# Scores ahead of the hash steps, a split first tile, and an expert that waits block by block

## What is computed

```python
q_bits = (np.einsum('bhsd,dk->bhsk', q, proj) > 0)
k_bits = (np.einsum('bhsd,dk->bhsk', k, proj) > 0)
mask = q_bucket[:, :, :, None] == k_bucket[:, :, None, :]
scores = np.where(mask, scale * np.matmul(q, k.transpose(0, 1, 3, 2)), -1000000000.0)
attn = softmax(scores)          # minus the row's maximum, exp, divided by the row's sum
x = attn @ v                    # then 768 x 512
...
expert_idx = np.argmax(x @ w_gate, axis=1)       # 8 experts, at most 192 tokens each
h = np.maximum(np.einsum('ecd,edf->ecf', disp, w1), 0.0)
y = np.einsum('ecf,efd->ecd', h, w2)             # times the gate's weight
...
h = x @ w_in                                     # 512 -> 2048
out = (h * np.tanh(softplus(h))) @ w_out
```

## Time and profile before

| what | value |
|---|---|
| median of the runs | 420.18 us (419.67 to 420.54) |
| the profiled execution | 420.03 us, its span 418.2 us |
| PE busy | 402.1 us (96%) |
| DVE, ACT, POOL busy | 251.2, 200.5, 81.2 us |
| chain that ended last | PE 78%, DVE 13%, ACT 5%, issue 2%, DMA 1% |
| attention; experts; last network | 0 to 147 us; 158 to 280 us; 280 to 418 us |

### The profile page before, as it was taken

How to read it: one execution, slowest core, us unless ns; L and a number is a source line. 1 busy time by engine, 2 the same in 40 slices (tenths; PEclk the granted TensorE clock), 3 DMA queues, 4 the chain that set the end, 5 groups by cost and what they waited for, 6 DMA issues and landing times.

```text
span 418.2 us, 7265 instructions
## 1 busy us (share of the span) xinstructions
PE 402.1 (96%) x2675; PEld 369.2 (88%) x2677; DVE 251.2 (60%) x442; ACT 200.5 (48%) x388; POOL 81.2 (19%) x79
## 2 busy tenths in 40 slices
PE   8888999999999899999999999999999999999995
PEld 3567998998999788999999999999989899889984
DVE  4878889889999451201111011118899999777771
ACT  5867968968879311211011101106758564554441
POOL 1630320320600042084742600000000000000005
PEclk9999999999999989999999999999999999999999
DMA  8763931991600044999899899820000000000003
GB/s 297 251 126 87 267 75 39 303 201 40 239 2 0 2 162 148 407 388 320 302 380 344 327 371 350 330 92 2 0 2 0 2 2 2 0 0 2 0 2 150
DMA packets 15451, 62.85 MB, mean 150 GB/s; under 512 B 2112, under 2 KB 2752, under 8 KB 11328
## 3 DMA queue, kind: packets, MB, share of 16 engines
q1 hardware_dynamic: 14032, 58.51, 41.4%
q0 software_dynamic: 960, 3.15, 2.0%
q10 hardware_dynamic: 432, 0.83, 0.5%
HBM read 49.89 MB, written 3.15 MB: 127 GB/s over the span
## 4 chain that ended last, share of the span: by engine, by line
PE 78%; DVE 13%; ACT 5%; issue 2%; DMA 1%; POOLq 0%; POOL 0%; SPq 0%; DVEq 0%; ACTq 0%
PE ps L714 14%; PE ps L730 14%; PE ps L803 13%; PE ps L778 12%; PE ps L622 5%; PE ps L649 5%; PE ps L532 4%; DVE ptl L1160 3%; DVE nmax L1103 3%; PE ps L541 2%; PE ps L606 2%; PE ps L691 2%; PE ps L495 2%; ACT pth L926 1%; ACT prob L888 1%
## 5 line engine op out<-in xcount | busy, mean ns | idle before, releaser
L714 PE MATMUL ps<-xs,ring 128*128 x512 | 60.3, 278 | 1.9 <-issue 1.0
L714 PEld LDWEIGHTS ps<-xs,ring 128*128 128x128 f32 x512 | 58.6, 191 | 3.6 <-issue 3.5
L730 PE MATMUL ps<-hs,ring 128*128 128x128 f32 (+1 forms) x512 | 59.2, 276 | 0.0
L730 PEld LDWEIGHTS ps<-hs,ring 128*128 128x128 f32 x512 | 58.5, 192 | 0.0
L926 ACT ACTIVATE pth<-ps 128x384 fp32r<-128x384 f32 x96 | 42.2, 495 | 19.8 <-PE ps L649 19.3
L1160 DVE TENSOR_TENSOR ptl<-ps,pth 128x384 fp32r<-128x384 f32 x96 | 48.9, 551 | 3.6 <-ACT pth L926 3.5
L1103 DVE TENSOR_REDUCE nmax<-ps 128x1 f32<-128x768 f32 x48 | 45.7, 955 | 7.4 <-PE ps L532 5.9
L532 PE MATMUL ps<-ops 128*128 128x384 f32 x192 | 44.1, 352 | 1.4 <-ACT prob L888 1.4
L888 ACT ACTIVATE prob<-ps,nmax 128x768 f32<-128x768 f32 x48 | 43.5, 907 | 3.1 <-DVE nmax L1103 3.1
L649 PE MATMUL ps<-cfs,prob 128*128 128x128 f32 x288 | 41.3, 276 | 2.3 <-DVE ptl L1160 2.0
L778 PE MATMUL ps<-yh,wih 128*128 128x384 f32 x128 | 43.0, 336 | 0.3 <-ACT hc L1004 0.3
(11 more groups left out here) (160 smaller groups left out, 688.4 us busy)
## 6 DMA issues: line engine op xcount, KB each, us to landing
ring<-in_w SPq DMA_DIRECT2D x32, 1024.0 KB, 6.8
winraw<-in_w_in SPq DMA_DIRECT2D x8, 512.0 KB, 5.9
woutraw<-in_w_out SPq DMA_DIRECT2D x8, 512.0 KB, 6.7
ops<-kh SPq DMA_DIRECT2D x12, 192.0 KB, 3.5
ops<-qh SPq DMA_DIRECT2D x6, 384.0 KB, 5.7
xg<-rows SPq DMA_DIRECT2D x1, 1539.0 KB, 8.7
raw<-in_vt SPq DMA_DIRECT2D x4, 384.0 KB, 5.2
raw<-in_qt SPq DMA_DIRECT2D x3, 384.0 KB, 6.7
```

The lines of the kernel that those rows point to most:

```text
L714: last = mm(ps[:, fc // 2, (fc % 2) * WIDE:(fc % 2) * WIDE + W], wa[:, 2 * fc // KF, kd, P * (fc % (KF // 2)):P * (fc % (KF // 2)) + P], x ...
L730: last = mm(ps[:, 4 + half * KD // 2 + k, 0:W], wb[:, half, fc, P * k:P * k + P], hs[:, fc, 0:W], start=(fc == 0), stop=(fc == KF - 1))
```

## The change

It has three parts. On PE, `prepare("A", n)` is moved from the front of a unit to behind the scores of unit n + 2. The scores of the very first unit are issued in two pieces: those of QA and KA ahead of the one-hot matmuls, in place of two matmuls of zeros, and those of QB and KB where all four stood; the six matmuls of zeros ahead of these write bank 5 and no longer bank 0, which now holds sums. In the expert loop the copies of the sorted blocks count on xa and xd and no longer on Ha and Hd, so the first expert waits block by block; POOL sets Ha and Hd to their start values with two more memsets, and ACT and DVE no longer wait for one another ahead of the loop.

```diff
@@ -129,7 +129,7 @@
         col = {n: place(n, [P, NT], F32) for n in
                ("mx", "km", "sum", "sume", "gate", "slot", "pos", "gk")}
         bounds = place("bounds", [P, E, 2], I32)
-        mark = place("mark", [P, 2], F32)
+        mark = place("mark", [P, 4], F32)
         toki = place("toki", [P, NT], U32)
         sloti = place("sloti", [P, NT], U32)
         rows = nc.dram_tensor("rows", [T, DM + 1], F32, kind="Internal").ap()
@@ -439,8 +439,10 @@
             gp.wait_ge(s["opsB"], DMASB * (NPAIR - 1))
             gp.wait_ge(s["pd"], PD * (NPAIR - 1))
             gp.wait_ge(s["vs"], NPAIR)
-            nc.gpsimd.memset(mark[:, 0:1], 0.0).then_inc(s["xa"], TURN)
-            nc.gpsimd.memset(mark[:, 1:2], 0.0).then_inc(s["xd"], TURN)
+            nc.gpsimd.memset(mark[:, 0:1], 0.0).then_inc(s["xa"], 1)
+            nc.gpsimd.memset(mark[:, 1:2], 0.0).then_inc(s["xd"], 1)
+            nc.gpsimd.memset(mark[:, 2:3], 0.0).then_inc(s["Ha"], 2)
+            nc.gpsimd.memset(mark[:, 3:4], 0.0).then_inc(s["Hd"], 2)
             nc.gpsimd.memset(yh[:, :, :].bitcast(F32), 0.0).then_inc(s["ya"], 2)
             nc.gpsimd.memset(yl[:, :, :].bitcast(F32), 0.0).then_inc(s["yd"], 2)
             gp.wait_ge(s["g"], 1)
@@ -523,16 +525,17 @@
                 mm(ps[:, bank, 0:HALF], c16(name)[0:HROWS, :], bits[0:HROWS, c, :], start=True,
                    stop=True).then_inc(s["ao"], 1)
 
-            def scores(n):
+            def scores(n, sides=((QA, KA), (QB, KB))):
 
                 o = ops[:, (n // NT) % 4, :, :]
                 u, b = n % NT, n % 2
-                for a, kk in ((QA, KA), (QB, KB)):
+                for a, kk in sides:
                     for c in range(2):
                         last = mm(ps[:, 2 * b + c, 0:HALF], o[:, a, P * u:P * u + P],
                                   o[:, kk, c * HALF:c * HALF + HALF], start=(a == QA), stop=(a == QB),
                                   skip_group_check=True)
-                last.then_inc(s["S"], 1)
+                if (QB, KB) in sides:
+                    last.then_inc(s["S"], 1)
 
             def keep_clock(count, bank=OB):
 
@@ -547,16 +550,15 @@
             pe.wait_ge(s["pja"], 2)
             head_hash(0, (4, 5))
             pe.wait_ge(s["c"], 16)
+            scores(0, ((QA, KA),))
             for c in range(2):
                 pe.wait_ge(s["ab"], c + 1)
-                if c == 0:
-                    keep_clock(2, 0)
                 head_onehot(c, "headk", 2 + c)
                 head_onehot(c, "headq", 6 + c)
-            keep_clock(6, 0)
+            keep_clock(6, 5)
             pe.wait_ge(s["ak"], 2)
             pe.wait_ge(s["aq"], 2)
-            scores(0)
+            scores(0, ((QB, KB),))
             scores(1)
 
             def x_free():
@@ -628,7 +630,6 @@
                     last.then_inc(s["PV"], 1)
 
             for n in range(UNITS):
-                prepare("A", n)
                 pe.wait_ge(s["P"], n + 1)
 
                 u = n + 2
@@ -641,6 +642,7 @@
                         pe.wait_ge(s["opsB"], DMASB * (u // PER))
                     scores(u)
 
+                prepare("A", n)
                 if n == 0:
                     pe.wait_ge(s["c0"], 16)
                 for b in range(2):
@@ -939,15 +941,13 @@
                    scale=col["gk"][:, t:t + 1]).then_inc(s["xga"], 1)
             for kd in range(0, KD, 2):
                 act.wait_ge(s["perm"], kd + 1)
-                av(xs[:, kd, 0:WIDE], ps[:, 4 + kd, 0:WIDE], ACT.Copy).then_inc(s["Ha"], 1)
+                av(xs[:, kd, 0:WIDE], ps[:, 4 + kd, 0:WIDE], ACT.Copy).then_inc(s["xa"], 1)
 
 
             act.wait_ge(s["bnd"], 1)
             act.wait_ge(s["zy"], 1)
             act.wait_ge(s["xga"], NT // 2)
             act.wait_ge(s["xgd"], NT // 2)
-            act.wait_ge(s["Ha"], 2)
-            act.wait_ge(s["Hd"], 2)
             with act.Fori(0, E) as e:
                 st, n_e = load_bounds(act, e)
 
@@ -977,7 +977,7 @@
                                ACT.Copy).then_inc(s["xa"], 1)
                         else:
                             av(xs[:, b, 0:P * 4], ps[:, b, :],
-                               ACT.Copy).then_inc(s["xa"], 1 if b == 0 else TURN * (E - 2) + 1)
+                               ACT.Copy).then_inc(s["xa"], 2 if b == 0 else TURN * (E - 2) + 1)
 
 
             def split_in(f):
@@ -1223,15 +1223,13 @@
                                 co["gk"][:, t:t + 1], None, ALU.mult).then_inc(s["xgd"], 1)
             for kd in range(1, KD, 2):
                 dve.wait_ge(s["perm"], kd + 1)
-                V.tensor_copy(xs[:, kd, 0:WIDE], ps[:, 4 + kd, 0:WIDE]).then_inc(s["Hd"], 1)
+                V.tensor_copy(xs[:, kd, 0:WIDE], ps[:, 4 + kd, 0:WIDE]).then_inc(s["xd"], 1)
 
 
             dve.wait_ge(s["bnd"], 1)
             dve.wait_ge(s["zy"], 1)
             dve.wait_ge(s["xga"], NT // 2)
             dve.wait_ge(s["xgd"], NT // 2)
-            dve.wait_ge(s["Ha"], 2)
-            dve.wait_ge(s["Hd"], 2)
             with dve.Fori(0, E) as e:
                 st, n_e = load_bounds(dve, e)
 
@@ -1261,7 +1259,7 @@
                                           ps[:, 5, :].rearrange("p (k c) -> p k c", k=2)).then_inc(s["xd"], 1)
                         else:
                             V.tensor_copy(xs[:, b, 0:P * 4],
-                                          ps[:, b, :]).then_inc(s["xd"], 1 if b == 1 else TURN * (E - 2) + 1)
+                                          ps[:, b, :]).then_inc(s["xd"], 2 if b == 1 else TURN * (E - 2) + 1)
                     dve.wait_ge(s["back"], 16)
                     V.tensor_copy(toki[:, :], xg[:, :, DM]).then_inc(s["tokw"], 1)
```

## The result

The changed kernel took 415.45 us in the median of 4 runs (415.22 to 416.30), the kernel before 419.93 in the same comparison: a ratio of 0.9897, with a 95% interval of 0.9876 to 0.9918. A second comparison with more runs of the kernel before (6 and 13 runs) gave 0.992 (0.9891 to 0.9948), 416.36 against 418.97. So the two comparisons put the change at 4.5 and 2.6 us. Their intervals overlap, and a part of what follows is on what moved the two medians apart. The profiled execution took 415.41, its span is 413.6.

The account below looks back on a forecast made before the run. The prediction took the kernel to be bound by a chain of waits, 78% of it PE and 13% DVE. Its terms 1.4 + 1.4 + 0.8 = 3.6 off 420.03 gave a forecast of 416.5 us, range 415.2 to 419.0.

Parts of the forecast that it names:

- The start: From the start to unit 2's exponential: splitting the first scores was to gain 1.4 us in all.
- The 0.55: At the start, PE's queue ahead of the first row maximum was to shorten by 0.55 us, bounds 0.36 and 0.79.
- The forecast on the copy L408: At the start, DVE's `q_low(1)`, ready at 13.15, was to wait for POOL's running copy until 13.30.
- The rival in which POOL keeps its turn: At the start, POOL's subtraction gets in ahead of DVE; start gives 0 to 0.5, time 417.4 to 417.9; chance 0.2.
- the 1.1 for `q_low(1)`: At the start, the length in us taken for DVE's `q_low(1)` with nothing in its way.
- Units 4 and 6: In attention, scores issued ahead of PE's waits were to gain 1.4 us, bounds 0.7 and 1.75.
- my upper bound of 1.75: In attention units 4 and 6, the most that could be gained: PE's own lead, 1.75 us.
- The rival in which ACT eats the lead: From unit 4 to 8, ACT and DVE eat PE's lead; with another short gain, 417.5 to 419.2; chance 0.14.
- The first expert: At the first expert's entry, PE's idle 0.83 was to go by waiting for block 0 alone; gain 0.8 us.
- My upper bound 0.83: At the first expert's entry, the gain was priced at 0.63 to 0.83 us, the whole of PE's idle time.
- The cap of 0.9 from the reload: Behind the first expert, the reload landing at 172.25 was to let at most about 0.9 us of lead past.
- The clock: Rival: half clock falls on sorting or expert matmuls; with 10 us of it the kernel takes 421.5; chance 0.03.

Follow-up runs that it names:

- with the zeros: Kernel before and changed kernel, each with five matmuls of zeros added in PE's waits at the end of attention: 418.88 and 415.77 us.
- e2_order: Kernel before with only `prepare("A", n)` moved behind the scores: 417.40 us, ratio 0.9954.
- e3_expert: Kernel before with only the block by block wait of the first expert: 418.48 us, ratio 0.9977.
- e10_beforefill: Kernel before with five matmuls of zeros added in PE's waits at the end of attention: 418.88 us, ratio 0.9992.
- e5_nosplit: Changed kernel without the split of the first unit's scores, two matmuls of zeros back: 415.90 us, ratio 0.992.
- e7_fill: Changed kernel with five matmuls of zeros added in PE's waits at the end of attention: 415.83 us, ratio 0.9917.
- e6_allb: Changed kernel with all six hash tasks of the second pair at the back of units 3 to 8: 417.10 us, ratio 0.9935.
- r_after: The changed kernel run again, unaltered, beside the kernel before: 416.36 us against 418.97, ratio 0.992.
- e4_vlater: Kernel before with only POOL's copy and subtraction of v moved between its subtractions for k and q: 420.27 us, ratio 1.0024.

## Why the prediction was right, and where not

Forecast were 416.5 us and 3.6 off; measured were 415.45 and 4.5, later 416.36 and 2.6. Sorted by the clock as in the table, the two kernels' medians lie 3.6 apart (418.78 and 415.22) and 3.4 (419.83 and 416.41), with the zeros 3.0 and 2.7. The direction and the size were right, and 415.45 lies in the range but only 0.25 above its lower end; some of its steps and its sum need a word.

- *The start.* The 0.55 ahead of the first row maximum was 0.54 in the profile, 0.48 of it between the second bits (8.44) and the row maximum, where it took 3.34 before and 2.86 after; the rest is that the bits came earlier. That `q_low(1)` would then run ahead of POOL's subtraction, and the exponential of unit 2 start 1.5 earlier, came true (1.6), and in the profile the start gave 1.3 of the forecast 1.4. What failed is to take that for each execution: the step "POOL's times hang on transfers ... which the change leaves alone" is true, but these transfers land at another time in each execution. In the profiles of e2_order, e3_expert and e10_beforefill, whose start is that of before, the subtraction came second and `q_low(1)` took 1.29, 1.30 and 0.96. How much the collision costs shows between the first row maximum and that of unit 5: 12.96 in the profile of before and 13.01 in e5_nosplit, and 12.20 to 12.22 in the eleven others that leave POOL's order alone, with the split or without. So the split gives about 0.5 and, in the executions that had the collision, 0.8 more. The five profiles with the old start and POOL's old order have it twice, the eight with the split never. My 1.4 read one profile's luck as the kernel's habit.
- *The forecast on the copy L408.* I took it that DVE waits for it. It does in e7_fill, and in e6_allb the copy waits for DVE (both below). In the changed kernel's profile only 0.07 of it was left. The rival in which POOL keeps its turn came in no profile with the split. And the 1.1 for `q_low(1)` was too long: with nothing in its way it took 0.96.
- *Units 4 and 6.* The term was mis-sized: 1.4 forecast, 1.76, 1.75 and 1.80 measured (changed kernel, e2_order, e5_nosplit), which is my upper bound of 1.75 and a little over. I let ACT be late from unit 6 on and PE wait 0.3 at unit 8. In the profile after there is no such wait. The prediction doesn't print the adding up of ACT's steps; I had put the read of the sum behind each exponential (0.20) in it as time of its own, but the copy behind it starts 0.87 after the exponential did, beside the read (35.18, 35.96 and 36.05 above). The rival in which ACT eats the lead falls with it.
- *The first expert.* 0.8 forecast, 0.9 measured, in the changed kernel and in e3_expert. PE's loop entry had no cost of its own that the rows show. My upper bound 0.83 was too low, since PE without the wait also overlaps its first matmul with the sorting: it starts at 154.12, and the sorting's modelled end is 154.29. The cap of 0.9 from the reload didn't bind. In the changed kernel's profile the reload landed at most 7.3 after its issue; in e3_expert and r_after it took 8.7 and 8.6 as before, was issued at 162.52 and 159.94, and so still landed 0.9 before the transposes (172.09 and 169.47).
- *The clock.* I had it as a rival on the slower side only, and in the first comparison it was on the other side. Three of the changed kernel's four executions had full clock through the gating by the line above, and its profile is 0.74 ahead there of the profile of before, which had the half clock. That is most of the 0.9 by which 4.5 exceeds 3.6; the clocks of the four timed executions of before are not on record, so this is likely and not shown. The half clock isn't a part of either kernel but of the execution, and there is no sign that the change alters how often it comes: 5 of 10 executions against 36 of 65.
- *The sum.* What the change itself gives is 0.48 + 1.76 + 0.90 = 3.1, and 0.8 more where the old start would have had the collision. The forecast 3.6 lies between the two, so it fits the medians at equal clock because a start that was too high (1.4) and a term that was too low (1.4 for units 4 and 6) partly cancelled, which is luck. And 420.03 less 3.6, with 0.15 on it, is 416.6 and not 416.5.

## What to carry to other kernels

A wait in front of an engine's queue holds all that is queued behind it: put what needs no wait ahead of the instruction that does, and the lead stays if the other engines have room. When a gain rests on which of two engines comes first, look at more than one profile, since a transfer's landing can turn it. A difference under 1% is read between executions with the same granted clock. And before a step is moved back out of a wait, follow its results to their last reader: with the last codes one unit later 0.7 us was gained here, with them two units later it was all lost.

## What the runs showed of the hardware

In these traces DVE's subtraction with both inputs in SBUF, the on-chip buffer, and POOL's instructions that read SBUF don't run side by side: whichever starts first finishes in its usual time, and the other's grows by what was left of the first, all but 0.13 to 0.14 us of it. In e7_fill the copy was first (the subtraction's line is 1075 there, two lines were added above it), in e6_allb DVE was, by 0.04 us:

```profile
13.14 0.82 POOL L408 CAST vs<-raw 128x768 fp32r<-128x768 f32 x1
13.23 1.55 DVE L1075 SCALAR_TENSOR_TENSOR ops<-qq,ops 64x768 fp32r<-64x768 f32 x1
```

```profile
12.67 0.96 DVE L1073 SCALAR_TENSOR_TENSOR ops<-qq,ops 64x768 fp32r<-64x768 f32 x1
...
12.71 1.61 POOL L408 CAST vs<-raw 128x768 fp32r<-128x768 f32 x1
```

Alone they take 0.96 and 0.82. In e7_fill 0.73 of the copy was left when DVE started, and DVE took 0.59 longer; in e6_allb 0.92 was left of DVE's, and the copy took 0.79 longer. The Trainium skill ("SBUF — State Buffer", section "Who interferes with whom") says that the order of issue and not the kind of operation decides who blocks; by that rule the runs agree, in both orders. It is not a matter of the copy having one input: it blocked and was blocked like the subtraction. Nor does it take two inputs on DVE's side: the 128x3 instruction of e4_vlater above has one, and it ended 0.03 after POOL's subtraction did.
